# First MLP beside attention: other starts for its tiles, other places for its maximum, exponential, SoLU and square, two sets of bias buffers

## The reference

```python
scores = q @ k.T / sqrt(64)                      # 32 heads, 576 x 576
cum = cumsum(maximum(s, 0)); bias = -(cum[:, None] - cum[None, :])
scores = where(causal, -1e9, scores + minimum(bias, 0))
attn = softmax(scores); x = (attn @ v)           # -> 2304 x 512

h = x @ w_in                                     # 512 -> 1024
e = exp(h - max(h)); sm = e / (sum(e) + 1e-9)
solu = h * sm; mu = mean(solu); var = mean((solu - mu) ** 2)
x = ((solu - mu) / sqrt(var + 1e-6) * g_ln) @ w_out   # 1024 -> 512

h = x @ w_in2                                    # 512 -> 2048
out = (h * clip(h + 3, 0, 6) / 6) @ w_out2       # 2048 -> 512
```

## Time and profile before

| | |
|---|---|
| median of 3 runs | 921.59 us (917.24, 921.59, 922.11) |
| the profiled execution | 918.19 us, its span 916.4 us |
| PE busy, PEld busy | 845.5 us (92%), 750.7 us (82%) |
| DVE, ACT, POOL busy | 441.9 us (48%), 412.8 us (45%), 296.5 us (32%) |
| mean granted clock of PE | 0.976 |
| `exp_row`, L1132, mean | 580 ns, and 191 ns to read its sum |
| chain that ended last | PE 69%, DVE 10%, ACT 9%, issue 5%, POOL 4%, DMA 2% |

### The profile page before, as it was taken

One profiled execution on the slowest core, in us unless ns is written; L12 is line 12 of the kernel. 1 busy time (PEld: TensorE's weight loads), 2 busy tenths in 40 slices (PEclk: granted clock), 3 DMA queues, 4 the chain that ended last, 5 costly groups with the idle time before them and its releaser, 6 DMA issues.

```text
span 916.4 us, 13790 instructions
## 1 busy us (share of the span) xinstructions
PE 845.5 (92%) x4916; PEld 750.7 (82%) x4916; DVE 441.9 (48%) x1061; ACT 412.8 (45%) x911; POOL 296.5 (32%) x391
## 2 busy tenths in 40 slices
PE   7778779989899998999898999999999999999997
PEld 5566668888688887888787999989898999999996
DVE  3747767776676767667455232232322232332222
ACT  6745766657566566555223243232322232322222
POOL 7764466455644465453165253000000000000000
PEclk9789879999999999999999999999999999999999
DMA  7536434334434344331402040000000000000000
GB/s 232 176 111 208 119 97 141 96 99 125 124 95 115 91 115 123 108 113 40 137 2 92 1 138 1 35 1 1 35 0 1 35 1 1 35 1 1 35 1 34
DMA packets 39426, 66.84 MB, mean 73 GB/s; under 512 B 4480, under 2 KB 16512, under 8 KB 39360
## 3 DMA queue, kind: packets, MB, share of 16 engines
q1 hardware_dynamic: 39360, 65.97, 23.7%
HBM read 61.16 MB, written 4.79 MB: 72 GB/s over the span
## 4 chain that ended last, share of the span: by engine, by line
PE 69%; DVE 10%; ACT 9%; issue 5%; POOL 4%; DMA 2%; SPq 0%; DVEq 0%; ACTq 0%; POOLq 0%
PE psum L794 9%; PE psum L843 7%; PE psum L845 7%; PE psum L861 7%; PE psum L844 7%; PE psum L862 7%; PE psum L860 7%; PE psum L761 4%; PE psum L823 3%; PE psum L736 3%; ACT prob L1132 3%; ACT p_hi L1155 2%; DVE es L1018 2%; PE psum L807 2%; PE psum L722 2%
## 5 line engine op out<-in xcount | busy, mean ns | idle before, releaser
L1086 DVE SCALAR_TENSOR_TENSOR act<-act,psum 128x384 f32<-128x384 f32 x96 | 53.2, 554 | 286.8 <-ACT act L1240 286.8
L1240 ACT ACTIVATE act<-psum,three 128x384 f32<-128x384 f32 x96 | 55.9, 582 | 285.7 <-PE psum L845 285.7
L843 PE MATMUL psum<-x_hi,w_hi 128*128 128x384 f32 x384 | 129.5, 337 | 0.9 <-DVE x_lo L1044 0.9
L845 PE MATMUL psum<-x_hi,w_lo 128*128 128x384 f32 x384 | 129.5, 337 | 0.0
L844 PE MATMUL psum<-x_lo,w_hi 128*128 128x384 f32 x384 | 129.0, 336 | 0.0
L862 PE MATMUL psum<-w_hi,g_lo 128*128 128x512 f32 x288 | 113.9, 395 | 0.0
L861 PE MATMUL psum<-w_lo,g_hi 128*128 128x512 f32 x288 | 113.7, 395 | 0.0
L860 PE MATMUL psum<-w_hi,g_hi 128*128 128x512 f32 x288 | 112.0, 389 | 0.0
L953 DVE TENSOR_TENSOR p_lo<-psum,p_hi 128x512 fp32r<-128x512 f32 (+2 forms) x128 | 71.9, 572 | 79.5 <-ACT p_hi L1155 79.0
L1155 ACT ACTIVATE p_hi<-psum 128x512 fp32r<-128x512 f32 (+2 forms) x128 | 62.3, 500 | 96.0 <-PE psum L736 63.1
L610 POOL TENSOR_TENSOR qk_hi<-qk_raw,qk_hi 64x256 fp32r<-64x256 f32 (+1 forms) x64 | 57.0, 891 | 125.3 <-ACT qk_hi L1124 124.1
(11 more groups left out here) (95 smaller groups left out, 1881.6 us busy)
## 6 DMA issues: line engine op xcount, KB each, us to landing
qk_raw<-qk SPq DMA_DIRECT2D x32, 480.0 KB, 3.5
qk_raw<-qk SPq DMA_DIRECT2D x32, 256.0 KB, 2.7
bias<-cum_dram SPq DMA_DIRECT2D x32, 256.0 KB, 3.9
v_raw<-v_rows SPq DMA_DIRECT2D x32, 160.0 KB, 3.1
bias_tail<-cum_dram SPq DMA_DIRECT2D x32, 144.0 KB, 3.8
out<-out_sb SPq DMA_DIRECT2D x6, 768.0 KB, 3.5
w_raw<-w_in SPq DMA_DIRECT2D x16, 256.0 KB, 3.2
w_raw<-w_out SPq DMA_DIRECT2D x16, 256.0 KB, 4.1
```

Source lines behind the costliest of these rows:

```text
L843: pe.matmul(ps, w2_hi[f][:, cols], xh, start=(c_ == 0), stop=False)
L845: last = pe.matmul(ps, w2_lo[f][:, cols], xh, start=False, stop=(c_ == NC - 1))
```

## The change

- `STARTS`: tiles start at other slots. The first at 14 (12 before), then 25 (21), 33 (31), 39 (37), 45 (44), 54 (51), 60 (59), one slot later each up to tile 9, at the same slots for tiles 10 to 12, and one to two later from tile 13 on; the end is 135 (133). `FIRST_STEP` follows, as do X_AT and the splits.
- DVE: `max1` stands right behind `row_max` in part 3, `solu` there in part 5 (was at the end of part 4); part 4's `copy_x2` stands behind `scale_pair`.
- ACT: `exp1` and `square` stand behind `copy_corr` instead of at the head of the slot; the weight splits stand behind `split_qk`.
- `square` writes a buffer of its own in SBUF, `squares`; where PE waited for the square before it reused the banks of `h`, it waits for `solu`.
- `bias` has two buffers for each e, one for each kind of unit, with a semaphore of its own for the second kind; a load waits for the last user of its own place (`bias_before`), and the first of the second kind (unit 4) is issued at slot 1.
- The scratch memory for DMA descriptors is 4096 bytes.

```diff
-STARTS = [12, 21, 31, 37, 44, 51, 59, 65, 71, 77, 84, 90, 96, 102, 109, 115, 121, 127, 133]
+STARTS = [14, 25, 33, 39, 45, 54, 60, 66, 72, 78, 84, 90, 96, 103, 110, 116, 122, 129, 135]
...
+def bias_place(u):
+
+    return u % 2 if FIRST_KIND[u] else 2
+
+
+def bias_before(u):
+
+    return max([m for m in range(u) if bias_place(m) == bias_place(u)], default=-1)
...
-        bias = [sb(a_region, f"bias{p}", [P, BANK]) for p in range(2)]
+
+        bias = [[sb(a_region, f"bias{p}{c}", [P, BANK]) for c in range(2)] for p in range(2)]
...
+        squares = sb(first, "squares", [P, F1])
...
             def load_bias(u, e):
-                before = user_before(u)
+                before = bias_before(u)
...
                 for u in range(2, UNITS):
                     for e in range(2):
-                        before = user_before(u)
-                        if BASE[before] + (e if FIRST_KIND[before] else 2 * e + 1) == n + 1:
+                        before = bias_before(u)
+                        if before < 0:
+                            if n == max(1, BASE[u] - 8):
+                                load_bias(u, e)
+                        elif BASE[before] + (e if FIRST_KIND[before] else 2 * e + 1) == n + 1:
                             load_bias(u, e)
...
-                before = n - 2 if n <= FIRST_STEP else n - 1
+                before = max([m for m in range(n) if turn(m) == turn(n)], default=-1)
...
-                    wait(pe, sq_done, t - 1 if t >= NT - 2 else t)
+                    wait(pe, solu_done, t - 1 if t >= NT - 2 else t)
...
                         row_max(n + 1, tile, e, col)
+                if r == 3:
+                    max1(t)
+                if r == 5:
+                    solu(t)
                 if r == 0 and t >= 3:
                     copy_x2(2 * (t - 3) + 1)
                 if 0 <= n < ITEMS:
                     split_probs(n)
+                if n in SCALES_AT:
+                    scale_pair(SCALES_AT[n])
                 if r == 4 and t >= 2:
                     copy_x2(2 * (t - 2))
-                if n in SCALES_AT:
-                    scale_pair(SCALES_AT[n])
...
-                if r == 3:
-                    max1(t)
-                if r == 4:
-                    solu(t)
...
-                sc.activation(h_of(t), es[:, :], ACT.Square, bias=neg_mu[:, p:p + 1],
+                sc.activation(squares[:, :], es[:, :], ACT.Square, bias=neg_mu[:, p:p + 1],
...
-                if r == 4:
-                    exp1(t)
-                if r == 5:
-                    square(t)
                 if 0 <= n < ITEMS:
                     copy_probs(n)
...
                 for u, e in SUMS_AT.get(n, ()):
                     copy_corr(u, e)
+                if r == 4:
+                    exp1(t)
+                if r == 5:
+                    square(t)
...
-    nc = bacc.Bacc("TRN2", target_bir_lowering=False, num_devices=1)
+    nc = bacc.Bacc("TRN2", target_bir_lowering=False, num_devices=1, dynamic_dma_scratch_size=4096)
```

More of the change, by code:

```diff
@@ L77 @@
 P_COLS = 2 * HEAD_P + P
-A_WORDS = 4 * DH + 6 * ST + 6 * NQ * DH + 2 * BANK + SEQ + 3 * P + BANK + NQ * P + 2 * P_COLS
+A_WORDS = 4 * DH + 6 * ST + 6 * NQ * DH + 4 * BANK + SEQ + 3 * P + BANK + NQ * P + 2 * P_COLS
 PJW = 2 * P
 NPJ = NC * (NT // 2)
-STARTS = [12, 21, 31, 37, 44, 51, 59, 65, 71, 77, 84, 90, 96, 102, 109, 115, 121, 127, 133]
+STARTS = [14, 25, 33, 39, 45, 54, 60, 66, 72, 78, 84, 90, 96, 103, 110, 116, 122, 129, 135]
 STEPS = 6
@@ L369, in build @@
         v_loaded = [[sem(f"v_loaded{p}{i}") for i in range(2)] for p in range(2)]
-        bias_loaded = [[sem(f"bias_loaded{p}{i}") for i in range(2)] for p in range(2)]
+        bias_loaded = [[sem(f"bias_loaded{p}{i}") for i in range(3)] for p in range(2)]
         bias_tail_loaded = sem("bias_tail_loaded")
@@ L456, in bias_loads @@
         def bias_loads(u):
-            return len(units_of_half(u)) - (1 if half_of(u) == half_of(0) else 0)
+            return sum(bias_place(m) == bias_place(u) for m in range(1, u + 1))
         def tokens(u):
@@ L485, in load_bias @@
                 h = head_of(u, e)
-                sp.dma_start(bias[e][:, at:at + n], cum_dram[h:h + 1, 0:n].to_broadcast([P, n])).then_inc(bias_loaded[e][half_of(u)], 16)
+                sp.dma_start(bias[e][kind(u)][:, at:at + n], cum_dram[h:h + 1, 0:n].to_broadcast([P, n])).then_inc(bias_loaded[e][bias_place(u)], 16)
             def load_bias_tail(u):
@@ L834, in hidden2 @@
                 if j == 0:
-                    pe.wait_ge(sq_done, NT - 1)
+                    pe.wait_ge(solu_done, NT - 1)
                     pe.wait_ge(pT_lo_done, LOS_BEFORE[ITEMS])
@@ L851, in output @@
                     if g == 0:
-                        pe.wait_ge(sq_done, NT)
+                        pe.wait_ge(solu_done, NT)
                         pe.wait_ge(lnT_lo_done, 2 * NT)
@@ L936, in row_max @@
                     else:
-                        dve.wait_ge(bias_loaded[e][half_of(u)], 16 * bias_loads(u))
+                        dve.wait_ge(bias_loaded[e][bias_place(u)], 16 * bias_loads(u))
                     b_at = u % 2 * CUT if FIRST_KIND[u] else 0
-                    b = bias[e][:, b_at:b_at + w]
+                    b = bias[e][kind(u)][:, b_at:b_at + w]
                 wait(dve, pT_ready, max([m + 1 for m in range(n) if (ITEM[m][1] % 2, ITEM[m][1] == 4) == (k % 2, k == 4)],
@@ L1166, in copy_bias @@
                 sc.wait_ge(bias_spread, e + 1)
-                sc.activation(bias[e][:, 0:CUT], bank(H_BANK + e, CUT), ACT.Copy).then_inc(bias_copied, 1)
+                sc.activation(bias[e][1][:, 0:CUT], bank(H_BANK + e, CUT), ACT.Copy).then_inc(bias_copied, 1)
             def split_w_in(i):
@@ L1233, in _ @@
                         copy_bias(1)
+                if W_OUT_FROM <= n < W_OUT_FROM + NF1:
+                    split_w_out(n - W_OUT_FROM)
+                if t == NT - 1 and r in (1, 2, 4, 5):
+                    split_x2(0, (1, 2, 4, 5).index(r))
                 if 0 <= n - W_IN_FROM < W_IN_PARTS:
```

## The result

The changed kernel takes 889.80 us (median of 4 runs, 887.97 to 890.87), the one before beside it 921.84 us (917.24 to 922.11): a ratio of 0.966 (95%: 0.963 to 0.970), 32 us less. Its profiled execution took 890.87 us (span 889.1), 27.3 less than the profiled one of before.

The account below looks back on a forecast made before the run. PE was taken as the bound, its idle time as what can be won; -16.5 + 2.5 + 2 - 6 - 4 - 3 + 2 = -23 from 918.2 gave 895, plus half of 3.4 made 897 us; range 883 to 912.

Parts of the forecast that it names:

- The sum of -23: All terms for the whole kernel, taken from the profiled 918.2 us to give 895 for its like.
- Starts, -16.5 + 2.5 + 2 = -12: Other tile starts: -16.5 for xs_lo waits and their clock; +2.5 two more bare steps before tile 2; +2 low clock there.
- The four waits: PE's waits for xs_lo, input of the first MLP's hidden layer: 3.77, 2.95, 3.56 and 2.42 us, 12.7 in all.
- Steps 12, 31 and 59: Sign that the forecast is right: these steps, at old starts of tiles 0, 2 and 6, last under 5 us.
- bare: A step without MLP work: 2.35 us (step 14), set by the chain transposes, p_hi on ACT, p_lo on DVE, next transposes.
- The orders, -6 - 4 - 3 + 2 = -11: DVE and ACT orders: -6 x2's copy, -4 middle prob, p_lo and nmax waits, -3 early, +2 SoLU ahead of split_probs.
- The price of +2: Part 5 steps of 12 tiles: SoLU ahead of split_probs is hidden by only 0.3 us; +2 us (0 to +15).
- The -3 early: Early stretch: square behind the attention's work and later SoLU take 3 us off the 16.5 of prob and nmax waits.
- Data, 0: Squares into SBUF, two sets of bias buffers (bounds -1 and +1), smaller DMA scratch: no effect on time.
- rival (b): Five bare steps before tile 2 keep PE's clock low into tile 2; up to 6 us more, 902 us; chance 0.11.
- my mark for (b): Sign against the forecast, for rival (b): the clock from 90 to 130 us is under 0.7.
- the 2.42 of tile 15: PE's wait for xs_lo at tile 15's start, 2.42 us; its later start was to save all 2.4.

Follow-up runs that it names:

- run 1: Also written starts_only: the kernel before with the new STARTS and nothing else; 907.56 us, ratio 0.985.
- run 10: Also written w_out_later: the changed kernel with DVE's part of the second weight's split one slot later than ACT's part; 884.58 us, ratio 0.960.
- run 2: The kernel before with all new places of calls on DVE and ACT, old STARTS, square still into PSUM and waited for; 907.51 us, ratio 0.985.
- run 7: The changed kernel with solu alone back at the end of part 4; 895.12 us, ratio 0.972.
- run 4: The changed kernel with DVE's old order (max1, solu, x2's copy), ACT's order kept new; 902.61 us, ratio 0.979.
- run 5: The changed kernel with ACT's old order (exp1 and square at the head of the slot), DVE's kept new; 912.48 us, ratio 0.992.
- run 3: The kernel before with only the bias buffers, squares in SBUF, waits for SoLU and small DMA scratch; 917.52 us, ratio 0.996.
- run 8: The changed kernel with 16 small unused matmuls at the end of PE's slots 10 to 13 and 28 to 32; 886.69 us, ratio 0.963.
- changed_again: The changed kernel unaltered, measured once more as base for later runs; 889.46 us, ratio 0.965.
- run 11: The changed kernel with SoLU of tiles 0 and 1 behind split_probs, and the last tile's a slot earlier; 891.79 us, ratio 0.968.

## Why the prediction was right, and where it was not

The range (883 to 912), the direction and the division into starts and orders held; 897 was 7.2 above the median. Step by step:

**The base.** The sum of -23 started from the profiled 918.2, and I added half of the 3.4 us to the median. In four sets of runs before's median was 919.7 to 921.8, so its profiled execution was among the shortest; the other half, 1.7 us, was missing.

**Starts, -16.5 + 2.5 + 2 = -12.** Measured alone, -13.3 (run 1). The four waits went as written, 12.7 to 0.8. Steps 12, 31 and 59 of the changed kernel:

```profile
47.35:50.13 2.78, 2.42 (x8) 1.61 (x9) 2.35 (x5) 1.36 (x4) 2.70 (x3) 0.50 0.80 225
111.65:117.70 6.05, 2.37 (x18) 1.96 (x18) 4.81 (x18) 4.86 (x12) 4.05 (x6) 0.82 0.65 193
217.29:221.12 3.83, 3.83 (x36) 3.79 (x35) 3.29 (x11) 3.23 (x9) 3.49 (x6) 1.00 0.36 114
```

Steps 12 and 59 are under 5 us, from 9.22 and 9.40 in the earlier trace rows. Step 31 is not: 6.05 us for 2.37 of PE's work. I had taken it as bare and 3.6 us long; it carries SoLU of tile 1 and a weight split, one behind the other on DVE (the rows of run 10), and PE waits 3.6 us for `p_lo`.

**The orders, -6 - 4 - 3 + 2 = -11.** Measured -13.4 alone (run 2) and -17.8 on top of the starts, data included (907.56 to 889.80). x2's copy gave 4.5 in the middle (7.3 to 2.8), not 6. `prob`, `p_lo` and `nmax` gave 6.9 at the same items (8.9 to 2.0), not 4. The price of +2 for SoLU ahead of `split_probs` in twelve full part 5 steps was not there: PE's idle time in those steps of tiles 2 to 13 fell from 5.5 to 0.0 us in all, as in the timeline of tile 12. The -3 early was not there either: up to item 33 the orders gave 0.5 us on top of the starts, `prob` fell by 2.0 and `p_lo` rose by 4.2. In steps 29 to 32 they cost 1.0 (16.95 in starts_only, 17.94), in steps 21 to 24 they gave 1.9 (14.0, 12.1). SoLU's new place is not what costs there: with SoLU back at the end of part 4 (run 7) these steps take 18.9 and 14.1 us, although PE's wait of 3.6 us for `p_lo` stands right behind the new place.

My account named ACT's order as the cause and DVE's as its cost. Runs 4 and 5 show that most of the gain needs both: ACT's alone gives 5.0 of the 17.8 us, DVE's alone loses 4.9. ACT's idle time in the changed kernel:

```profile
L1204 ACT ACTIVATE squares<-es,neg_mu 128x1024 f32<-128x1024 f32 x18 | 20.7, 1149 | 14.7 <-DVE neg_mu L1038 14.6
L1198 ACT ACTIVATE es<-psum,nmax 128x1024 f32<-128x1024 f32 x18 | 19.9, 1106 | 8.0 <-DVE nmax L1025 7.9
```

Ahead of the square it was 37.0 us and is 14.7, ahead of the exponential 26.5 and now 8.0; nearly all that is left, 13.7 and 7.9, lies behind the start of item 111, where no later `copy_probs` can be held up. Up to there the two kinds of wait behind which attention work is queued are (us):

| | ACT, for `neg_mu`, ahead of the square | DVE, for the exponential, ahead of SoLU |
|---|---|---|
| before | 27.1 | 0 |
| DVE's order alone (run 5) | 43.0 | 0 |
| ACT's order alone (run 4) | 0 | 6.3 |
| both | 0.9 | 0 |

**Data, 0.** Measured -3.4, outside my bounds, cause open (run 3). The square into SBUF takes 1149 ns against 1118 into PSUM. The Trainium skill (ScalarE: Activation LUTs, Step-by-step: what each stage is for) has PSUM as the faster target; the trace agrees, by 31 ns or 0.6 us in 18 squares, off the chain.

**The clock, rival (b).** It is 0.71 from 104 to 128 us, but 0.83 from 90 to 130, where my mark for (b) was under 0.7. Its price is about 3 us by run 8, not clear of the noise, where I had 2 in the sum and up to 6 more in the rival.

**The end.** From item 111's transposes on, 479.7 us before and 481.5 after (479.9 in changed_again, the same code). In it are the 2.42 of tile 15 gained, a part or two of MLP work that the later starts moved there, and 1.7 more for `x_lo` that I did not see: SoLU of the last tile comes a slot later, and the second MLP waits for that tile. Run 11 puts 1.6 us on it (479.9 to 478.3).

The rest of the 7 us: 1.7 the base, about 2.4 the orders alone (13.4 to 11), 1.3 the starts, 3.4 the data; these make 8.8, and I can't part them more finely, as single medians move by 1 to 2 us.

## What to carry to other kernels

Two in-order queues that hand work to each other are reordered together: a producer moved back with its consumer left in front turned 18 us of gain into 5 us of loss (run 5), and the same mechanism made run 11 a loss. Whether a call may stand ahead of the critical one is read from the matmuls of that very step: in the full steps there were 0.7 us of cover. In a bare one PE stalled 3.6 us behind the same call; yet a wait right behind a call is not what the call costs, as these steps were longer with SoLU at either other place (18.9 us in run 7 and 20.4 in run 11, against 17.9 for steps 29 to 32). Where one engine waits for a piece made in the same slot by another, a slot of distance is cheap and worth trying first; here it gave 4.9 us (3.5 of them found in the steps that it can touch), more than holding the clock up did.

## What the runs showed of the hardware

Low clocks in stretches where PE waits don't fall at the same place in each execution, though the code before them is the same: step 13 lasted 4.67 us at a clock of 0.57 in the changed kernel and 3.13 at 1.00 in w_out_later, step 23 4.40 at 0.61 and 3.19 at 1.00 in the same two, step 33 5.54 at 0.66 in the changed kernel and 6.80 at 0.52 in changed_again, the same code. Such a step is worth 1 to 2 us, as much as most single edits here, so that effects of under 3 us were read from medians and not from one profile.
